# Phase one of an attention and two-expert kernel, unrolled in a new order: part of batch 0 ahead, then expert groups of 256, 320 and 288 tokens among all other heads

## The reference, cut to what matters

```python
# q, k, v: 4 batches x 8 heads x 576 positions x 64
scores = scale * np.matmul(q, k.transpose(0, 1, 3, 2))
mask = block_i >= block_j                 # blocks of 64 positions
scores = np.where(mask, scores, -1000000000.0)
attn = np.exp(scores - scores.max(-1)); attn = attn / (attn.sum(-1) + 1e-09)
x = np.matmul(attn, v)                    # rearranged to 2304 tokens x 512
h = np.maximum(np.maximum(x @ w1, x @ w2), x @ w3)     # 512 -> 768
y = h @ w_out                                          # 768 -> 512
h = y @ w_in; out = (h * np.cos(h)) @ w_out2           # 512 -> 2048 -> 512
```

## Time and profile before

| what | value |
|---|---|
| median of 3 runs (lowest, highest) | 1024.53 us (1023.39, 1025.28) |
| span of the profiled execution | 1023.5 us |
| TensorE busy | 953.7 us, 93% |
| VectorE busy | 664.8 us, 65% |
| ScalarE busy | 559.4 us, 55% |
| GpSimd busy | 185.5 us, 18% |
| batch 0's heads alone | up to 131.4 us |
| three passes of eight periods | 131.4 to 528.1 us |
| groups of batch 3, then phase two | from 528.1 us |

### The profile page before, as it was taken

How to read it: one execution, slowest core, us unless ns; L and a number is a source line. 1 busy time by engine, 2 the same in 40 slices (tenths; PEclk the granted TensorE clock), 3 DMA queues, 4 the chain that set the end, 5 groups by cost and what they waited for, 6 DMA issues and landing times.

```text
span 1023.5 us, 16894 instructions
## 1 busy us (share of the span) xinstructions
PE 953.7 (93%) x5760; PEld 870.1 (85%) x5760; DVE 664.8 (65%) x1247; ACT 559.4 (55%) x1249; POOL 185.5 (18%) x166
## 2 busy tenths in 40 slices
PE   3876699999999999999999998999999999999998
PEld 2765599889899989889999997779999999999996
DVE  5899977576675776757721137777757657576564
ACT  4566544455445545445423336666666656566665
POOL 4443322122121221212115412220000000000000
PEclk8567689999999999999999999999999999999999
DMA  6423211211220312102011322101010010100000
GB/s 215 123 84 99 54 53 31 72 41 37 78 59 26 86 30 82 50 27 64 2 65 59 120 69 72 59 21 62 1 62 0 0 61 0 33 29 0 31 1 31
DMA packets 47476, 53.41 MB, mean 52 GB/s; under 512 B 23216, under 2 KB 30512, under 8 KB 47408
## 3 DMA queue, kind: packets, MB, share of 16 engines
q1 hardware_dynamic: 47408, 52.51, 17.0%
HBM read 43.06 MB, written 9.44 MB: 51 GB/s over the span
## 4 chain that ended last, share of the span: by engine, by line
PE 37%; DVE 6%; ACT 6%; issue 2%; DMA 1%; SPq 0%; POOL 0%; ACTq 0%
PE S_ps L594 3%; PE S_ps L593 3%; PE S_ps L592 3%; DVE rest L749 2%; PE M_ps L566 2%; PE O_ps L566 2%; PE O_ps L564 2%; PE M_ps L564 2%; PE M_ps L565 2%; PE O_ps L565 2%; PE M_ps L517 2%; PE M_ps L519 2%; PE M_ps L518 2%; ACT whole L920 2%; ACT turns L915 2%
## 5 line engine op out<-in xcount | busy, mean ns | idle before, releaser
L517 PE MATMUL M_ps<-x,w_h 128*128 (+1 forms) x576 | 176.4, 306 | 0.8 <-ACT y_out L875 0.5
L518 PE MATMUL M_ps<-x,w_l 128*128 (+1 forms) x576 | 170.2, 295 | 0.0
L519 PE MATMUL M_ps<-x,w_h 128*128 (+1 forms) x576 | 170.0, 295 | 0.0
L852 ACT ACTIVATE pt_h<-T_ps 128x512 fp32r<-128x512 f32 (+1 forms) x128 | 62.7, 500 | 112.7 <-PE T_ps L467 112.4
L941 ACT ACTIVATE away<-rest 128x384 f32<-128x384 f32 x96 | 50.4, 525 | 115.2 <-DVE rest L749 115.2
L640 DVE TENSOR_SCALAR prob<-prob,inv_sum 128x128 f32<-128x128 f32 (+4 forms) x160 | 112.4, 767 | 1.1
L517 PEld LDWEIGHTS M_ps<-x,w_h 128*128 128x128 f32 x576 | 108.7, 189 | 4.4 <-ACT y_out L875 0.7
L518 PEld LDWEIGHTS M_ps<-x,w_l 128*128 128x128 f32 x576 | 108.7, 189 | 0.0
L519 PEld LDWEIGHTS M_ps<-x,w_h 128*128 128x128 f32 x576 | 108.5, 188 | 0.0
L467 PE MATMUL T_ps<-ident,prob 128*128 128x128 f32 (+2 forms) x480 | 80.0, 297 | 29.6 <-DVE prob L640 29.6
L647 DVE TENSOR_TENSOR pt_l<-T_ps,pt_h 128x512 fp32r<-128x512 f32 (+1 forms) x128 | 70.8, 567 | 47.5 <-ACT pt_h L852 45.6
(11 more groups left out here) (98 smaller groups left out, 2410.8 us busy)
## 6 DMA issues: line engine op xcount, KB each, us to landing
q_raw<-qT SPq DMA_DIRECT2D x64, 144.0 KB, 2.9
k_raw<-kT SPq DMA_DIRECT2D x64, 144.0 KB, 3.0
w_raw<-w_out SPq DMA_DIRECT2D x22, 256.0 KB, 2.6
w_raw<-w SPq DMA_DIRECT2D x12, 384.0 KB, 3.9
y_d<-y_out SPq DMA_DIRECT2D x32, 144.0 KB, 1.8
y_raw<-y_d SPq DMA_DIRECT2D x6, 768.0 KB, 4.6
out<-o_out SPq DMA_DIRECT2D x18, 256.0 KB, 2.2
v_raw<-v SPq DMA_DIRECT2D x32, 128.0 KB, 2.7
```

Source lines behind the costliest of these rows:

```text
L517: mm(o, w_h, x_h, start=k == 0, stop=False)
L518: mm(o, w_l, x_h, start=False, stop=False)
L519: last = mm(o, w_h, x_l, start=False, stop=k == KM - 1)
```

## The change

Phase one is written out for 33 periods without a loop (`early` and `walk`), and five things change in it.

1. **Early part.** Queries 0 to 255 of the eight heads of batch 0 (row tiles 0 and 1, called "A") run alone first, from their own tiles `qe_s`, `ke_h`, `ke_l`, `ve_s`, loaded and split four heads at a time. They are normalised as before.
2. **Chunks.** Batch 0 is cut in chunks of 256 and 320 tokens, the rest stays at 288. The 22 groups of the first chunk run in periods 0 to 8 among the remaining 320 queries ("B") of batch 0's heads; chunk two runs in periods 9 to 16, the other four in periods 17 to 32. The last 44 groups stay at the end.
3. **Order in a period.** The scores are now in three sets, A (tiles 0, 1), C (tile 3) and D (tiles 2, 4). D shares PSUM with A and C, so the scores D of a head wait for the exponentials of A and C.
4. **Normalisation of heads in `walk`.** `prob` is no longer multiplied. The inverted sums go to HBM (`inv_out`, 640 elements of 4 bytes) and come back copied on 64 partitions (`inv_in`), and x is multiplied once for a pair of heads (`take`).
5. **Buffers.** q and k of two heads are held, and raw weights land in the place of their low parts, so their loads wait for no ring. k of a head is loaded over `k_l`.

```diff
-PERIOD = ["scores0", "turn0", "G", "turn1", "exp0", "G", "G", "scores1", "turn2", "exp1", "G", "turn3",
-          "norm", "split", "G", "values0", "G", "values1", "take", "split_v", "load"]
-G_SLOTS = [6, 6, 6, 6, 5, 5, 6, 4]
+SCORES = {"A": (0, 1), "C": (3,), "D": (2, 4)}
+CHUNKS = [(0, 0, CUT), (0, CUT, S - CUT)] + [(b, c * S // 2, S // 2) for b in range(1, B) for c in range(2)]
+PERIOD = ["sA", "sC", "inv_out", "tA", "tB0", "eA", "G", "eC", "tB1", "G", "sD", "tB2", "inv_in", "G", "vA", "vB", "load_v",
+          "eD", "G", "split", "take", "norm", "split_v", "load", "G"]
+G_SLOTS = [3, 2, 3, 2, 3, 2, 3, 2, 2] + [3, 3, 3, 2, 3, 3, 3, 2] + [6, 6, 6, 5, 5, 6, 6, 4] + [6, 6, 6, 6, 5, 5, 6, 4]
+W_EARLY = {4: 0, 5: 1, 6: 2}
+W_PERIOD = {0: range(3, 6), 1: range(6, 9), 2: range(9, N_P1)}
+def early(step):
...
+    for a in range(1, H + 2):
+        if a < H:
+            step("scores", a)
+        if a <= H:
+            step("turn", a - 1)
+        if a < H:
+            step("exp", a)
+        if a >= 2:
+            step("values", a - 2)
+        if a < H:
+            step("norm", a)
...
+            def inv_out(n):
+                sp.wait_ge(inverted, n + 1)
+                sp.dma_start(inv_d[n, :].rearrange("(t p) -> p t", p=P), inv_sum[:, n % 4, 0:NT],
...
+            def inv_in(n):
+                sp.wait_ge(inv_stored, 16 * (n + 1))
...
+            def scores(n, s):
+                pe.wait_ge(q_low, n + 1)
+                pe.wait_ge(k_low, n + 1)
+                if s == "D":
...
+                    pe.wait_ge(exped["C"], n + 1)
+                    if whole(n):
+                        pe.wait_ge(exped["A"], wholes(n))
...
+            def take(n):
...
+                dve.wait_ge(x_added, n + 1)
+                dve.wait_ge(inv_loaded, 16 * (n + 1))
+                V.tensor_tensor(x_f[:, q0:], x_f[:, q0:], inv_b[:, pair % 2, q0:], ALU.mult).then_inc(x_normed, 1)
```

More of the change, by code:

```diff
@@ L75, with whole, wholes @@
-PERIOD_LAST = ["turn0", "turn1", "G", "turn2", "turn3", "G", "values0", "values1", "take", "G", "G"]
-G_SLOTS = [6, 6, 6, 6, 5, 5, 6, 4]
-assert PERIOD_LAST.count("G") == G_SLOTS[-1]
-Y_PERIODS = {next(n + 1 for n in range(H) if sum(G_SLOTS[:n + 1]) > g): GROUPS[g][0]
-             for g in (NG // 2 - 1, NG - 1)}
+CUT = 2 * P
+N_MAIN = B * H
+EARLY_GROUP = 4
+def whole(n):
+    return n >= H
+def wholes(n):
+    return max(0, n + 1 - H)
+SCORES = {"A": (0, 1), "C": (3,), "D": (2, 4)}
+S_AT = {0: 0, 1: P, 3: BANK, 2: 0, 4: 3 * P}
@@ L125, in some, with walk @@
     return True
+def early(step):
+    step("split", 0)
+    step("scores", 0)
+    step("split_v", 0)
+    step("exp", 0)
+    step("norm", 0)
+    step("split", 1)
+    step("split_v", 1)
+    for a in range(1, H + 2):
[9 more added lines that the diff above has]
+            step("norm", a)
+        if a in W_EARLY:
+            step("weights", W_EARLY[a])
+def walk(step):
+    for n in range(N_MAIN + 1):
+        g = G_FIRST[n]
+        for name in period_steps(PERIOD if n < N_MAIN else PERIOD_LAST, G_SLOTS[n]):
+            if name == "G":
+                step("G", g)
+                g += 1
+            elif name[0] in "tvi" or name == "take":
+                if n > 0 and (whole(n - 1) or name not in ("tA", "vA")):
+                    step(name, n - 1)
+            elif name in ("split", "load_v"):
+                if n + 1 < N_MAIN:
+                    step(name, n + 1)
+            elif name == "load":
+                if n + 2 < N_MAIN:
+                    step(name, n + 2)
+            elif n < N_MAIN and (whole(n) or name not in ("sA", "eA")):
+                step(name, n)
+        if n in W_PERIOD:
+            for p in W_PERIOD[n]:
+                step("weights", p)
 def program(nc, qT, kT, v, w1, w2, w3, w_out, w_in, w_out2, ident_in, y_d, out):
@@ L515, in group @@
+                        x_h, x_l = (x[:, b % 2, part, k, t0:t0 + n] for part in range(2))
                         w_h = w123_h[:, j, k, f * P:(f + 1) * P]
@@ L709, in step @@
                 elif name == "norm":
-                    normalise(i, n)
-                elif name == "split":
-                    if not isinstance(i, int) or H * (i + 1) + n + 1 < B * H:
-                        q_split(i, n + 1)
+                    inverse(n)
                 elif name == "take":
-                    take(i, n)
-            def groups_of_last():
-                for g in range(NG):
-                    group(B - 1, g)
-            phase1(dve, first, step, groups_of_last)
+                    take(n)
@@ L724, in y_split @@
+            early(early_step)
+            q_split(0)
+            walk(step)
+            for g in range(G_FIRST[N_MAIN + 1], N_GROUPS):
+                group(g)
             def y_split(c, k):
@@ L854, in take @@
[L854 to L866 removed]
+                raw, hi, _, _ = piece(p)
@@ L1034, in step @@
                 elif name == "weights":
[L1035 to L1045 removed]
+                    split_weights(n)
@@ L1046, in _ @@
+            early(early_step)
+            k_split(0)
+            walk(step)
+            for g in range(G_FIRST[N_MAIN + 1], N_GROUPS):
+                group(g)
+                if of_last(g) >= 2 and of_last(g) % 2 == 0 and of_last(g) // 2 <= N_IN - N_P1:
+                    split_weights(N_P1 + of_last(g) // 2 - 1)
             for p in range(N_IN, len(PIECES)):
```

1135 lines of the change are left out of this document (639 added, 496 removed).

## The result

The changed kernel took 1090.05 us in the median of four runs (1088.01 to 1093.91), the kernel before 1024.9 us on the same chip: ratio 1.0648, 95% interval 1.0623 to 1.0673. The forecast had the sign, slower, but 1033 us; 65 us were added instead of 8.

What follows compares the result with a forecast made beforehand. It took one chain per period, not TensorE's work, to bound periods 0 to 16. 59 + 103 + 113 + 262 + 495.4 = 1032.4 us of span, 1033 as median, slower than before; own range 1027 to 1044, full range 1006 to 1049.

Steps and rivals of the forecast that it cites:

- periods 0 to 16: Heads beside chunks one and two: one chain per period; 103 and 113 us, with 168.5 work and 47.5 waits.
- periods 17 to 32: Remaining heads with four groups: TensorE's earlier work less one head's scores, 262 us; bounds 7 less and 8 more.
- The early part: Batch 0's A queries alone: scores C of head 0 at 59 us, 72 us earlier than before; +-6.
- the tail: Batch 3's 44 groups and phase two, after the periods: unchanged work and order, 495.4 us.
- rival one: Periods 0 to 16: TensorE stays the bound, waits W = 24 us, 1010 us in all; chance 0.31.
- Sums through HBM: Store and load of each head's inverted sums: 3.5 us taken, bounds 2 and 8, hidden in the period.
- Rival two: B periods: the sums' store takes 6.7 us, factors and v come late; 16 us more, 1049; chance 0.10.
- ScalarE's block at the fourth place: Periods 17 to 32: ScalarE held by a group costs some 2 us in two or three periods; counted as nothing.
- VectorE has five operations behind each second head's take: Periods 0 to 16: these operations meet the next maxima; 3.4 and 1.6 us added.
- TensorE's price of the transposes: Heads' TensorE work, estimated by columns and blocks: 6.3 us a head, part A 1.5 and part B 4.8.
- TensorE in periods 1 to 7 busy 80 to 90% at clock 1.00: Sign that the forecast is right: TensorE at full clock, waiting before scores C and D.
- rival three: B periods: waits keep TensorE's clock low, first nine periods 50 us more, 1083; sign clock under 0.8; chance 0.04.

Runs made afterwards that it cites:

- best5: best4 with the 64-row blocks last in each set of transposes; 1029.9 us, ratio 1.0061 to the kernel before.
- sums_free: The change with the store of the sums left out and factors read from an input (output not the reference's); 1080.52 us, ratio 1.0565.
- take_first: The change with split, take and inverse ahead of the group at the fourth place on ScalarE and VectorE; 1070.78 us, ratio 1.044.
- free_take: take_first with the sums' store left out and factors from an input (output not the reference's); 1047.14 us, ratio 1.021.
- best2: take_late with the three w_out pieces split behind periods 3 and 5 instead of 2; 1052.99 us, ratio 1.0272.
- best3: best2 with the sums of batch 0's heads stored in 128 pieces of 20 bytes; 1043.46 us, ratio 1.0182.
- split_first: The change with the next head's q and k split ahead of the fourth place's group, TensorE's order unchanged; 1087.63 us, ratio 1.0609.
- take_late: take_first with the multiply and split of an odd head's x one period later on VectorE; 1053.87 us, ratio 1.0297.
- best4: best3, but a batch's last head has its multiply and split of x at once; 1038.79 us, ratio 1.0139.
- warm: The change with 168 added matmuls of 256 columns, into the bank the next group overwrites, ahead of scores; 1098.82 us, ratio 1.0732.
- turn_last: The change with the 64-row blocks last in each set of transposes (only set B0 differs); 1087.74 us, ratio 1.0622.
- packed_store: The change with sums stored as 128 pieces of 20 bytes and copied rows read with a stride, in two operations; 1095.57 us, ratio 1.0699.
- sums_const: The change with factors read from an input without waiting for the store, which stays (output values meaningless); 1091.56 us, ratio 1.0661.

## Why the prediction was right in sign and wrong in size

| part | forecast | change | best5 |
|---|---|---|---|
| up to scores C of head 0 | 59 | 59.0 | 58.5 |
| periods 0 to 16 | 216 | 255.3 | 214.8 |
| periods 17 to 32 | 262 | 276.3 | 257.0 |
| batch 3's groups and phase two | 495.4 | 495.5 | 495.6 |

**Right.** The early part, by its end to 0.1 us and by its steps: first scores at 14.8 us (14), head 0 normalised at 18.8 (18), head 1 at 23.9 (22.3), head 7 at 52.4 (53); the tail; that chains and not TensorE set periods 0 to 16, so rival one (1010 us) is out; the sign. That best5 takes 214.8 us where 216 was forecast is partly chance: the forecast had 168.5 us of work and 47.5 of waits and counted ScalarE's block, best5 has 185.9 and 28.9 without that block.

**The step that failed most in periods 0 to 16: "Sums through HBM: each head adds a store of 640 elements of 4 bytes ... I take 3.5 ... Hidden, by 1.2 us in a B period".** The store took 8.3 us, past the upper bound of 8, which was three times a row of 256-byte runs. Rival two had the mechanism, at 6.7 us and 16 us in all. By runs: 9.5 us with the store out of the change (sums_free), 23.6 with it out of take_first (free_take), 9.5 still between best2 and best3. The order on ScalarE and VectorE counts for more over the whole (19.3 us by take_first, 33.4 from sums_free to free_take), but its block in periods 0 to 16 was in the forecast, and the store stood there at nothing. The Trainium skill (DMA: Bandwidth & Descriptors, Rules for kernel authors) has one descriptor an element for such a store. By 10.5 ns a packet, which the Trainium skill (DMA: Bandwidth & Descriptors, Measured) gives for loads issued from GpSimd, an estimate is 6.7 us for 640 and 1.3 for 128. The runs showed 8.3 and 1.4: here the Trainium skill was nearer than the row that I went by.

**"ScalarE's block at the fourth place gives some 2 us back in two or three periods ... at nothing".** It was paid in nearly every period: 10.9 us over heads 17 to 31 by split_first, 14.3 with take and inverse ahead too. The walk had looked at the split and not at x_low behind it.

**"VectorE has five operations behind each second head's take ... I add 3.4 and 1.6".** Moving the last three of an odd head a period on brought 16.9 us (take_late against take_first), with 10.1 gained in periods 8 to 16 and 12.8 in periods 0 to 7, and 5.7 lost in heads 17 to 31. With the factors late, or ScalarE late, all of them run into the next maxima.

**TensorE's price of the transposes.** I priced blocks by count. Before, the 64-row blocks stood last in each set (L467's loop sorts them), in the change B0 alternates. Undoing that brought 8.9 us from best4 to best5, with what the clock gave back in it, and 3.5 in heads 17 to 31, where the clock was at 1.00; in the change it brought 2.3 us in the whole.

**"TensorE in periods 1 to 7 busy 80 to 90% at clock 1.00", and rival three.** The clock was 0.82 and the engine 77% busy (85.28 of 111.24). Rival three had the low clock coming with idle gaps, and it came; its sign, a clock under 0.8 after 70 us, shows in the fourth slice of the row. The three longest waits end in three of its seven pieces, and two of these pieces begin inside such a wait. It adds to the delays above, by some 26 us at most, but isn't what starts them: in heads 17 to 31, at 1.00, the order of ScalarE and VectorE cost 14.3 us. How much of the 26 lengthened the periods is not shown; warm raised the clock and shortened periods 0 to 7 by 1.3 us only, with its fillers' own cost inside.

The delays do not add. Alone, split_first brought 2.4 us, sums_free 9.5, turn_last 2.3, and packed_store cost 5.5; best5 mends them all but the store of heads 8 to 31, with take, the weight pieces and the late half besides, and takes 60.2 less. GpSimd's subtractions cost period 3 6.8 us by its length (take_late against best2) and the whole 0.9; their own share of the total was not measured. Best5's work from 58.50 to 273.30 us is 185.9 us with 16.7 of it at the lower clock: by the same estimate as above 178 us at 1.00, as in the change (179), where 168.5 was forecast. So 18 of the 19 us between these two kernels can be the clock, and some 10 us of work were priced too low in both.

## What to carry to other kernels

When one chain per period sets the time, cost every engine's program order on it to the next period, with the operations that stand behind the one you look at; here a group's copy ahead of the split and of x_low on ScalarE counted as much as a DMA. Count a store of small pieces by their number, not by its bytes, and don't let one queue wait for its landing while later loads stand behind it. Where several delays have the same length, single edits measure little: take them away together before judging one.

## What the runs showed of the hardware

A store of 2.5 KB to HBM in 640 pieces of 4 bytes landed after 8.3 us, in 128 pieces of 20 bytes after 1.4 us. While such a store was under way, q's loads of 80 KB on the same queue took 6.9 instead of 2.5 us (sums_const).

VectorE's operations with both inputs in SBUF, and its tensor_scalar there, took 2.3 to 2.5 us each beside GpSimd subtractions of 2.4 us (0.16 to 0.49 without), while `x_f<-O_ps,x_low` with one input in PSUM and the reductions from PSUM kept their time. The Trainium skill (SBUF — State Buffer, Who interferes with whom) says that one of the two holds a shared port pair for its whole instruction and the other fully blocks; the trace agrees, as each length is that of one GpSimd instruction. In the earlier trace rows the same showed only as 5.66 against 1.70 us for five multiplies; at 97 us the cost went by the length of GpSimd's instruction: five elements a row took 2.30 us and 320 took 2.53.

The granted clock of TensorE stood at 0.50, its lower level, for 64.8 us between 58.96 and 314.30 us, in pieces of 6.8 to 13.7 us, and the waits of 4.6, 5.1 and 5.9 us end in three of them. A product of 256 columns took 0.41 us at 0.50 (the kernel before, 26.53 us) and 0.28 at 1.00. It took 0.41 too at 39.14 us in the change, where the windows read 1.00.
